# The order of the tiles in SBUF in a fused mLSTM, MLP and expert-mixture kernel

## The chip, the core and the metric

The program runs on one core of one Trainium2 chip. The metric is the device time of one execution in microseconds (us). A kernel's time is the median of several runs.

## The reference, cut to what matters

Three layers follow one another. 1,536 tokens (2 batches of 768) pass through an attention-like recurrence over 8 heads of 40 features, then through an MLP, then through 4 experts whose outputs are mixed by probabilities for each token.

```python
# layer 1: gated recurrence per head, y = o * (C q) / max(|n q|, 1)
x = attn_out.transpose(0, 2, 1, 3).reshape(1536, 320)
# layer 2: MLP, d_ff = 2048
h = x @ w_in
x = (h - np.tanh(h)) @ w_out
# layer 3: 4 experts, d_ff = 1024 each
for e in range(4):
    h = np.maximum(x @ w1[e], 0.0)
    out += p[:, e:e + 1] * (h @ w2[e])
```

## The kernel before

Each float32 operand of the two big layers is split into a high part of the type float32r and a low part, the rest that the high part leaves out. A product is then three matmuls (high by high, high by low, low by high). So the tiles come in pairs: `x_hi` and `x_lo` hold the activations with features on the partitions, `g_hi` and `g_lo` hold the hidden activations, and `w_all` holds both parts of 8 pieces of weights. `w_raw` is a ring of 3 slots in which the weights arrive by DMA. ScalarE writes the high parts, VectorE the low parts of activations, GpSimd the low parts of weights.

The main loop has 64 + 96 steps. Each step `m` does `up(m)` (features of x to a tile of 128 hidden features) and then `down(m - 1)`, so that TensorE works on one step while ScalarE and VectorE turn the result of the other into `g_hi` and `g_lo`.

- Steps 0 to 63 are the MLP: 4 groups of tokens with 256, 384, 384 and 512 tokens, 16 hidden tiles each. `up` is 8 matmuls (lines 1124 to 1128) with `w_all` stationary and `x_hi` or `x_lo` moving. `down_rows` is 8 matmuls (lines 1145 to 1147, twice, then 1153 and 1154) with `w_all` stationary and `g_hi` or `g_lo` moving. The attention of later chunks of 128 tokens is laid between these steps (lines 963 to 1011), with its own tiles: `feat` and `tok` (rings of inputs), `zb`, `fb`, `wa`, `state`, `spare`, and parts of `arena`. Chunks 5 to 11 send their sums through DRAM and read them back.
- Steps 64 to 159 are the experts: 4 experts, 3 groups of 512 tokens, 8 hidden tiles. `up` is the same 8 matmuls of 512 columns. `down_tokens` is 12 matmuls (lines 1174 to 1176, four times) of 320 columns, with `g_hi` or `g_lo` stationary and `w_all` moving. `out_acc`, a view of `arena`, gathers the mixed output, and 12 DMAs store it.

Tiles are placed in the order in which the code names them, one behind another, each at a multiple of 32 bytes. The build puts `w_all` at byte 16,512 of each partition, which is 258 times 64. All sizes up to `probs` are whole multiples of 64 bytes. `tok` has 3 x 968 floats, 11,616 bytes, which is 181.5 times 64. So in the kernel before, everything named behind `tok` begins 32 bytes past a multiple of 64: `feat` at 169,632, `zb`, `wa`, `fb`, `state`, `arena` at 197,600, `g_tmp` at 212,960, `g_hi` at 217,056, `g_lo` at 221,152 and `tails` at 225,248. The tiles ahead of it (`w_all`, `w_raw`, `x_hi` at 123,520, `x_lo`, `spare`, `ident`, `probs`, and `tok` itself at 158,016) begin at multiples of 64.

Of the kernel before, what the change touches and what calls it, by code (L numbers as in the profile page):

```python
# [6 lines left out]
F32R = mybir.dt.float32r  # L7
# [4 lines left out]
P = 128  # L12
BATCH, HEADS, SEQ, HD = 2, 8, 768, 40
D = HEADS * HD
TAIL = D - 2 * P
CH = P
CPB = SEQ // CH
STEPS = BATCH * CPB
TOK = BATCH * SEQ
HDE = HD + 1  # L20
QUAD = 4
PAIRS = HEADS // 2
# [4 lines left out]
RING = 3  # L27
# [19 lines left out]
ROWS = 64 + CPB * HEADS  # L47
# [15 lines left out]
GRP = 4 * CH  # L63
# [39 lines left out]
def mlstm_mlp_experts(nc, gates_d, tok_d, feat_d, w_d, probs_d, out_d):  # L103
    ctx = ExitStack()
    with ctx:
        def sb(name, shape, dt=F32):
            return ctx.enter_context(nc.sbuf_tensor(name, shape, dt))
# [3 lines left out]

        w_all = sb("w_all", [P, WARM, 2 * PIECE], F32R)
        w_raw = sb("w_raw", [P, RING, PIECE])


        x_hi = sb("x_hi", [P, 3, TOK], F32R)
        x_lo = sb("x_lo", [P, 2, TOK], F32R)
        spare = sb("spare", [P, 6 * P])  # L120
        yt = spare[:, 0:2 * D].rearrange("p (r d) -> p r d", d=D)

# [1 line left out]
        ident = sb("ident", [P, P])  # L124
        probs = sb("probs", [P, STEPS, EXPERTS])

        tok = sb("tok", [P, RING, 3 * D + HEADS])
        feat = sb("feat", [P, RING, 2 * PAIRS * CH])

        zb = sb("zb", [P, 2, HEADS, CH])  # L130

        wa = sb("wa", [P, 3, ROWS])

        fb = sb("fb", [P, PAIRS, CH])

        state = sb("state", [P, BATCH, PAIRS, 2, 64])

        dn = state[:, 0, 0, 1, 64 - HEADS:64]

        arena = sb("arena", [P, STEPS * D])  # L140
        dwork = arena[:, 0:1024].rearrange("p (q c) -> p q c", q=2)
        pwork = arena[:, 1024:3072].rearrange("p (r q c) -> p r q c", r=2, q=2)
        wv = arena[:, 3072:3728].rearrange("p (r h e) -> p r h e", r=2, e=HDE)
        beta = arena[:, 3728:3728 + ROWS]
        out_acc = arena[:, 0:STEPS * D].rearrange("p (n d) -> p n d", d=D)
        g_tmp = sb("g_tmp", [P, 2, GRP])
        g_hi = sb("g_hi", [P, 2, GRP], F32R)
        g_lo = sb("g_lo", [P, 2, GRP], F32R)
        tails = sb("tails", [P, 2, GRP])
        tail = tails[0:TAIL, :, :]  # L150


        early = g_tmp[0:ROWS, :, :].rearrange("p b c -> p (b c)")
# [1087 lines left out]
```

## Time and profile before

| | us |
|---|---|
| median of 3 runs | 598.75 |
| lowest and highest run | 597.57, 599.56 |
| the profiled execution, its whole time | 597.8 |
| its span, first to last instruction | 596.1 |
| TensorE busy in the span | 586.9 |
| VectorE, ScalarE, GpSimd busy | 237.2, 201.0, 104.1 |

The rows further down come from the profiled execution. Its whole time is 1.7 us more than its span. A matmul's recorded duration includes the time in which it overlaps with the next one, so the pace of TensorE is read from the distances between the starts of matmuls, not from durations.

### The profile page before, as it was taken

To read this page: it belongs to the slowest core of one execution; us is meant where nothing else is said; L and a number is where in the kernel's file an instruction comes from. 1 tells how busy PE (TensorE), PEld (TensorE's weight loads), DVE (VectorE), ACT (ScalarE), POOL (GpSimd) and SP (SyncE) were. 2 spreads that over 40 slices of the span, in tenths; PEclk is the share of its full clock that TensorE was granted. 3 is DMA by queue.
4 is the path that set the end of the run, shared out by engine and by line. 5 is a ranking of instruction groups with operands and counts; after the bars stand their busy time and mean duration, and the time that the engine had idled before them with its cause. 6 is when DMAs were issued, how large, how long until landed. Compare 5 with 4: busy or idle time off the path is not lost.

```text
span 596.1 us, 8943 instructions
## 1 busy us (share of the span) xinstructions
PE 586.9 (98%) x3660; PEld 531.9 (89%) x3660; DVE 237.2 (40%) x474; ACT 201.0 (34%) x396; POOL 104.1 (17%) x75
## 2 busy tenths in 40 slices
PE   8999999999999999999999999999999999999998
PEld 7899999989988888899999999999999999999997
DVE  6566757676655333413132313131323131323222
ACT  5675645555534444611113311113311111111111
POOL 3868201111000244420003400004400000000000
PEclk9999999999999999999999999999999999999999
DMA  6978544554220133210001210001000000001011
GB/s 252 347 241 279 221 111 134 169 158 112 58 50 27 38 98 104 93 58 0 1 1 48 98 49 1 1 1 48 1 0 1 2 0 1 1 0 45 1 44 46
DMA packets 35343, 43.84 MB, mean 74 GB/s; under 512 B 18670, under 2 KB 27878, under 8 KB 35302
## 3 DMA queue, kind: packets, MB, share of 16 engines
q1 hardware_dynamic: 35302, 43.26, 22.6%
q8 instruction: 29, 0.48, 0.3%
q14 instruction: 12, 0.10, 0.1%
HBM read 38.85 MB, written 4.40 MB: 73 GB/s over the span
## 4 chain that ended last, share of the span: by engine, by line
PE 90%; DVE 5%; issue 1%; DMA 1%; SPq 1%; ACT 1%; DVEq 0%
PE bank L1125 10%; PE bank L1126 10%; PE bank L1124 10%; PE bank L1175 9%; PE bank L1176 9%; PE bank L1174 9%; PE bank L1128 5%; PE bank L1127 5%; PE bank L1145 4%; PE bank L1147 3%; PE bank L1146 3%; PE bank L1153 1%; PE bank L1154 1%; PE bank L963 1%; PE bank L974 1%
## 5 line engine op out<-in xcount | busy, mean ns | idle before, releaser
L940 DVE SCALAR_TENSOR_TENSOR g_lo<-bank,g_hi 128x512 fp32r<-128x512 f32 x96 | 66.3, 691 | 254.2 <-ACT g_hi L659 254.2
L659 ACT ACTIVATE g_hi<-bank 128x512 fp32r<-128x512 f32 x96 | 57.5, 599 | 270.5 <-PE bank L1128 270.4
L1175 PE MATMUL bank<-w_all,g_hi 128*128 128x320 f32 x384 | 118.8, 309 | 0.0
L1176 PE MATMUL bank<-w_all,g_lo 128*128 128x320 f32 x384 | 118.6, 309 | 0.0
L1124 PE MATMUL bank<-x_hi,w_all 128*128 128x512 f32 (+2 forms) x318 | 117.2, 369 | 1.3 <-DVE x_hi L841 1.3
L1174 PE MATMUL bank<-w_all,g_hi 128*128 128x320 f32 x384 | 118.5, 309 | 0.0
L1126 PE MATMUL bank<-x_hi,w_all 128*128 128x512 f32 (+2 forms) x318 | 118.4, 372 | 0.0
L1125 PE MATMUL bank<-x_lo,w_all 128*128 128x512 f32 (+2 forms) x318 | 118.3, 372 | 0.0
L480 POOL TENSOR_TENSOR w_all<-w_raw,w_all 128x1408 fp32r<-128x1408 f32 x16 | 51.6, 3227 | 232.6 <-ACT w_all L542 232.6
L1175 PEld LDWEIGHTS bank<-w_all,g_hi 128*128 128x128 f32 x384 | 72.2, 188 | 3.8
L1174 PEld LDWEIGHTS bank<-w_all,g_hi 128*128 128x128 f32 x384 | 72.2, 188 | 3.7
L1176 PEld LDWEIGHTS bank<-w_all,g_lo 128*128 128x128 f32 x384 | 72.2, 188 | 0.0
L1126 PEld LDWEIGHTS bank<-x_hi,w_all 128*128 128x128 f32 x318 | 59.7, 188 | 8.9
L1124 PEld LDWEIGHTS bank<-x_hi,w_all 128*128 128x128 f32 x318 | 59.7, 188 | 7.5 <-DVE x_hi L841 2.0
L1125 PEld LDWEIGHTS bank<-x_lo,w_all 128*128 128x128 f32 x318 | 59.6, 188 | 6.0
L907 DVE TENSOR_TENSOR bank<-bank,g_tmp 128x384 f32<-128x384 f32 (+2 forms) x64 | 36.1, 564 | 66.0 <-ACT g_tmp L633 65.1
L1128 PE MATMUL bank<-x_hi,w_all 128*128 128x512 f32 (+2 forms) x160 | 59.0, 369 | 0.0
L1127 PE MATMUL bank<-x_hi,w_all 128*128 128x512 f32 (+2 forms) x160 | 58.9, 368 | 0.0
L633 ACT ACTIVATE g_tmp<-bank 128x384 f32<-128x384 f32 (+2 forms) x64 | 31.3, 490 | 70.8 <-PE bank L1128 70.2
L1145 PE MATMUL bank<-g_hi,w_all 128*128 128x384 f32 (+2 forms) x128 | 46.0, 359 | 2.9 <-DVE g_lo L921 2.8
L921 DVE TENSOR_TENSOR g_lo<-bank,g_hi 128x384 fp32r<-128x384 f32 (+2 forms) x64 | 35.4, 553 | 22.5 <-ACT g_hi L651 22.0
L1147 PE MATMUL bank<-g_hi,w_all 128*128 128x384 f32 (+2 forms) x128 | 43.4, 339 | 0.0
(134 smaller groups left out, 644.0 us busy)
## 6 DMA issues: line engine op xcount, KB each, us to landing
w_raw<-in_w SPq DMA_DIRECT2D x24, 704.0 KB, 4.1
feat<-in_feat SPq DMA_DIRECT2D x12, 512.0 KB, 4.7
tok<-in_tok SPq DMA_DIRECT2D x12, 484.0 KB, 5.6
zb<-z SPq DMA_DIRECT2D x10, 512.0 KB, 4.5
out<-arena SPq DMA_DIRECT2D x12, 160.0 KB, 1.9
spare<-xg SPq DMA_DIRECT2D x7, 256.0 KB, 2.6
fb<-f SPq DMA_DIRECT2D x14, 80.0 KB
xg<-feat SPq DMA_DIRECT2D x14, 80.0 KB
```

The lines of the kernel that those rows point to most:

```text
L659: A(g_hi[:, b, 0:N], h_ps[b][:, 0:N], ACT.Relu).then_inc(ghi_ready, 1)
L940: V.scalar_tensor_tensor(g_lo[:, b, 0:N], h_ps[b][:, 0:N], 0.0, g_hi[:, b, 0:N].bitcast(F32), ALU.max, ALU.subtract).then_inc(g_ready, 1)
L1124: mm(h, up_part(m, 0, k), x_hi[:, k, c], start=k == 0, stop=False)
L1125: mm(h, up_part(m, 0, k), x_lo[:, k, c], start=False, stop=False)
L1126: mm(h, up_part(m, 1, k), x_hi[:, k, c], start=False, stop=False)
L1127: mm(h, up_part(m, 0, 2), x_hi[:, 2, c], start=False, stop=False)
L1128: mm(h, up_part(m, 1, 2), x_hi[:, 2, c], start=False, stop=True).then_inc(h_ready, 1)
L1145: mm(out, high_w, high_g, start=first, stop=False)
L1147: mm(out, low_w, high_g, start=False, stop=stop)
L1174: mm(out, g_hi[:, b, t], high_w, start=first, stop=False)
L1175: mm(out, g_hi[:, b, t], low_w, start=False, stop=False)
L1176: last = mm(out, g_lo[:, b, t], high_w, start=False, stop=stop)
```

## The change

The calls that make the tiles are put in another order. `w_all`, `w_raw`, `x_hi` and `x_lo` stay where they are. Behind them come `g_tmp`, `g_hi`, `g_lo`, `tails` and `arena`, then `zb`, `feat`, `fb`, `state`, `spare`, `ident`, `probs` and `wa`, and `tok` is last. No instruction is added, taken away or moved; only the addresses of operands differ. From the sizes, `g_tmp` now begins at 154,240, `g_hi` at 158,336, `g_lo` at 162,432, `tails` at 166,528, `arena` at 170,624, `zb` at 185,984, `feat` at 194,176, `fb` at 206,464, `state` at 208,512, `spare` at 212,608, `ident` at 215,680, `probs` at 216,192, `wa` at 216,384 and `tok` at 217,728. All of these are multiples of 64.

```diff
         x_hi = sb("x_hi", [P, 3, TOK], F32R)
         x_lo = sb("x_lo", [P, 2, TOK], F32R)
-        spare = sb("spare", [P, 6 * P])
-        ident = sb("ident", [P, P])
-        probs = sb("probs", [P, STEPS, EXPERTS])
-        tok = sb("tok", [P, RING, 3 * D + HEADS])
-        feat = sb("feat", [P, RING, 2 * PAIRS * CH])
-        zb = sb("zb", [P, 2, HEADS, CH])
-        wa = sb("wa", [P, 3, ROWS])
-        fb = sb("fb", [P, PAIRS, CH])
-        state = sb("state", [P, BATCH, PAIRS, 2, 64])
+        g_tmp = sb("g_tmp", [P, 2, GRP])
+        g_hi = sb("g_hi", [P, 2, GRP], F32R)
+        g_lo = sb("g_lo", [P, 2, GRP], F32R)
+        tails = sb("tails", [P, 2, GRP])
         arena = sb("arena", [P, STEPS * D])
-        g_tmp = sb("g_tmp", [P, 2, GRP])
-        g_hi = sb("g_hi", [P, 2, GRP], F32R)
-        g_lo = sb("g_lo", [P, 2, GRP], F32R)
-        tails = sb("tails", [P, 2, GRP])
+        zb = sb("zb", [P, 2, HEADS, CH])
+        feat = sb("feat", [P, RING, 2 * PAIRS * CH])
+        fb = sb("fb", [P, PAIRS, CH])
+        state = sb("state", [P, BATCH, PAIRS, 2, 64])
+        spare = sb("spare", [P, 6 * P])
+        ident = sb("ident", [P, P])
+        probs = sb("probs", [P, STEPS, EXPERTS])
+        wa = sb("wa", [P, 3, ROWS])
+        tok = sb("tok", [P, RING, 3 * D + HEADS])
```

## Rows read from the trace of the kernel before

**Rows 1.** The page: TensorE's busy share, its granted clock, the chain by engine.

```profile
PE 586.9 (98%) x3660; PEld 531.9 (89%) x3660; DVE 237.2 (40%) x474; ACT 201.0 (34%) x396; POOL 104.1 (17%) x75
...
PEclk9999999999999999999999999999999999999999
...
PE 90%; DVE 5%; issue 1%; DMA 1%; SPq 1%; ACT 1%; DVEq 0%
```

**Rows 2.** Busy time by stretches: start, MLP without attention, experts, end.

```profile
core 0: us, PE busy (x) PEld busy (x) DVE busy (x) ACT busy (x) POOL busy (x), PEclk, DMA share, GB/s
0.00:19.50 19.50, 17.49 (x117) 14.67 (x117) 13.19 (x40) 10.08 (x20) 9.34 (x19) 0.91 0.72 265
...
214.00:249.70 35.70, 35.70 (x155) 28.84 (x155) 13.21 (x19) 18.06 (x25) 15.52 (x5) 1.00 0.31 101
...
400.00:592.00 192.00, 192.00 (x1070) 174.16 (x1069) 47.94 (x79) 36.84 (x57) 12.90 (x4) 1.00 0.03 11
592.00:596.10 4.10, 1.11 (x8) 0.85 (x6) 1.76 (x4) 0.00 (x0) 0.00 (x0) 1.00 0.47 160
```

**Rows 3.** TensorE's waits from 20 to 250 us: total, times, longest.

```profile
PE bank L1145 <- DVE g_lo L921: 2.8, 7, 1.3
PE bank L1124 <- DVE x_hi L841: 1.3, 2, 0.9
```

**Rows 4.** Timeline of TensorE, MLP steps of 256, 384, 512 columns: start, duration.

```profile
23.14 0.28 PE L1124 MATMUL bank<-x_hi,w_all 128*128 128x256 f32 x1
...
24.09 0.28 PE L1145 MATMUL bank<-g_hi,w_all 128*128 128x256 f32 x1
...
25.05 0.28 PE L1124 MATMUL bank<-x_hi,w_all 128*128 128x256 f32 x1
...
182.60 0.34 PE L1124 MATMUL bank<-x_hi,w_all 128*128 128x384 f32 x1
...
184.01 0.34 PE L1145 MATMUL bank<-g_hi,w_all 128*128 128x384 f32 x1
...
185.25 0.34 PE L1154 MATMUL bank<-g_lo,w_all 128*128 128x384 f32 x1
...
241.74 0.39 PE L1124 MATMUL bank<-x_hi,w_all 128*128 128x512 f32 x1
...
243.59 0.40 PE L1145 MATMUL bank<-g_hi,w_all 128*128 128x512 f32 x1
...
245.46 0.39 PE L1124 MATMUL bank<-x_hi,w_all 128*128 128x512 f32 x1
```

**Rows 5.** The same timeline, one expert step.

```profile
400.39 0.39 PE L1124 MATMUL bank<-x_hi,w_all 128*128 128x512 f32 x1
...
402.23 0.31 PE L1174 MATMUL bank<-w_all,g_hi 128*128 128x320 f32 x1
...
403.99 0.39 PE L1124 MATMUL bank<-x_hi,w_all 128*128 128x512 f32 x1
```

**Rows 6.** Groups of TensorE by shape: count, busy us, mean ns of one.

```profile
L1126 PE MATMUL bank<-x_hi,w_all 128*128 128x512 f32 x224 | 88.5, 395 | 0.0
...
L1145 PE MATMUL bank<-g_hi,w_all 128*128 128x512 f32 x32 | 12.8, 399 | 0.1
...
L1174 PE MATMUL bank<-w_all,g_hi 128*128 128x320 f32 x384 | 118.5, 309 | 0.0
```

**Rows 7.** Groups of VectorE, then of ScalarE, by shape (512 columns).

```profile
L921 DVE TENSOR_TENSOR g_lo<-bank,g_hi 128x512 fp32r<-128x512 f32 x16 | 11.1, 692 | 10.1 <-ACT g_hi L651 10.0
...
L876 DVE TENSOR_TENSOR x_lo<-bank,x_hi 128x512 fp32r<-128x512 f32 x2 | 1.3, 686 | 1.2 <-ACT x_hi L618 1.2
```

```profile
L651 ACT ACTIVATE g_hi<-bank 128x512 fp32r<-128x512 f32 x16 | 9.6, 600 | 11.6 <-DVE bank L907 11.5
...
L618 ACT ACTIVATE x_hi<-bank 128x512 fp32r<-128x512 f32 x2 | 1.1, 596 | 1.3 <-PE bank L1154 1.3
```

**Rows 8.** The page: DMA issues, count, KB each, us to landing.

```profile
w_raw<-in_w SPq DMA_DIRECT2D x24, 704.0 KB, 4.1
feat<-in_feat SPq DMA_DIRECT2D x12, 512.0 KB, 4.7
```

More of the change, by code:

```diff
@@ L119, in mlstm_mlp_experts @@
         x_lo = sb("x_lo", [P, 2, TOK], F32R)
-        spare = sb("spare", [P, 6 * P])
-        yt = spare[:, 0:2 * D].rearrange("p (r d) -> p r d", d=D)
-        xg = spare[:, :].rearrange("p (k g t) -> p k g t", k=3, g=2)
-        ident = sb("ident", [P, P])
-        probs = sb("probs", [P, STEPS, EXPERTS])
-        tok = sb("tok", [P, RING, 3 * D + HEADS])
-        feat = sb("feat", [P, RING, 2 * PAIRS * CH])
-        zb = sb("zb", [P, 2, HEADS, CH])
-        wa = sb("wa", [P, 3, ROWS])
-        fb = sb("fb", [P, PAIRS, CH])
-        state = sb("state", [P, BATCH, PAIRS, 2, 64])
-        dn = state[:, 0, 0, 1, 64 - HEADS:64]
+        g_tmp = sb("g_tmp", [P, 2, GRP])
+        g_hi = sb("g_hi", [P, 2, GRP], F32R)
+        g_lo = sb("g_lo", [P, 2, GRP], F32R)
+        tails = sb("tails", [P, 2, GRP])
+        tail = tails[0:TAIL, :, :]
         arena = sb("arena", [P, STEPS * D])
@@ L145, in mlstm_mlp_experts @@
         out_acc = arena[:, 0:STEPS * D].rearrange("p (n d) -> p n d", d=D)
-        g_tmp = sb("g_tmp", [P, 2, GRP])
-        g_hi = sb("g_hi", [P, 2, GRP], F32R)
-        g_lo = sb("g_lo", [P, 2, GRP], F32R)
-        tails = sb("tails", [P, 2, GRP])
-        tail = tails[0:TAIL, :, :]
+        zb = sb("zb", [P, 2, HEADS, CH])
+        feat = sb("feat", [P, RING, 2 * PAIRS * CH])
+        fb = sb("fb", [P, PAIRS, CH])
+        state = sb("state", [P, BATCH, PAIRS, 2, 64])
+        dn = state[:, 0, 0, 1, 64 - HEADS:64]
+        spare = sb("spare", [P, 6 * P])
+        yt = spare[:, 0:2 * D].rearrange("p (r d) -> p r d", d=D)
+        xg = spare[:, :].rearrange("p (k g t) -> p k g t", k=3, g=2)
+        ident = sb("ident", [P, P])
+        probs = sb("probs", [P, STEPS, EXPERTS])
+        wa = sb("wa", [P, 3, ROWS])
+        tok = sb("tok", [P, RING, 3 * D + HEADS])
         early = g_tmp[0:ROWS, :, :].rearrange("p b c -> p (b c)")
```

## The prediction

> **What bounds the kernel now.** I read the page first, then the busy time by stretches, then the waits of TensorE, and last single steps on the timeline. The page says that TensorE (PE) is busy for 586.9 of 596.1 us and that the chain which ended last is 90% TensorE; its clock is granted in full [rows 1]. The stretches say where the missing 9.2 us lie: 19.50 - 17.49 = 2.0 us in the start, 4.10 - 1.11 = 3.0 us in the end, none in the MLP without attention, none in the experts [rows 2]. What is left, 4.2 us, lies between 20 and 250 us, and two waits for VectorE make up 2.8 + 1.3 = 4.1 us of it [rows 3]. So the time is a sum of matmul paces, and the change can act in four places: the pace of a matmul whose moving operand is displaced, the pace of one whose stationary operand is, the small instructions of the other engines that lie on the chain, and DMAs.
>
> A busy TensorE hides its own losses, so the paces must come from starts. A step of the experts takes 403.99 - 400.39 = 3.60 us, of which 8 matmuls of `up` take 1.84 us (230 ns each for 512 columns) and 12 of `down_tokens` take 1.76 us (146.7 ns each for 320 columns) [rows 5]. At 2.4 GHz, the upper of the clock's two levels, 512 columns are 213.3 ns and 320 are 133.3 ns. So there are 17 and 13 ns on top, and if alignment were behind them, 96 steps of 20 matmuls would have about 27 us to give. The question is therefore whether the operands that are at 32 bytes past a multiple of 64 pay more than those that are not. The kernel before has both kinds side by side.
>
> **The change, part by part.**
>
> Moving operand. In `up` both operands are already at multiples of 64 (`w_all` stationary, `x_hi` and `x_lo` moving) and don't move. In `down_rows` the stationary one is `w_all`, and the moving ones are `g_hi` and `g_lo`, displaced by 32 bytes. The two stand in one step with equal columns. At 512 columns: 8 of `up` from 241.74 to 243.59, 231.3 ns each; 8 of `down_rows` to 245.46, 233.8 ns each, 2.5 more. At 384: 182.60 to 184.01, 176.3 ns; then 7 distances in 1.24 us, 177.1 ns, 0.8 more. At 256: 0.95 us, 118.8 ns; then 0.96 us, 120.0 ns, 1.2 more [rows 4]. Starts are given to 10 ns, so that each of these means is known to 1 ns or so. There are 16 tiles x 8 = 128 such matmuls in a group of tokens: 128 at 512 columns, 256 at 384, 128 at 256. If all of the difference is alignment, the change gives back 128 x 2.5 + 256 x 0.8 + 128 x 1.2 = 0.32 + 0.20 + 0.15 = 0.7 us. Recorded durations give a wider bound: 399 against 395 ns at 512 columns [rows 6], 4 ns, and with 4 ns for all 512 matmuls that is 2.0 us. The lower bound is nothing, since `down_rows` also differs in the banks that it writes. I take half of the 0.7 us, 0.35 us, because the differences are of the size of the rounding.
>
> Stationary operand. In `down_tokens` the moving operand is `w_all`, in place, and the stationary ones are `g_hi` and `g_lo`, displaced. No aligned matmul of 320 columns exists, so I compare with the line through the aligned ones: halfway between 118.8 ns at 256 and 176.3 ns at 384 is 147.5 ns [rows 4], against 146.7 ns measured [rows 5]. The displaced operand pays nothing; read the other way, putting it in place could cost 0.8 ns on each of 96 x 12 = 1,152 matmuls, 0.9 us. The other bound is the rounding of the comparison, 1 ns in favour of the change, 1.2 us. I take 0. The loads of the stationary operand are busy for 174.16 us of 192.00 beside the matmuls [rows 2], so a shorter load alone would lie beside other work; if it were longer than the matmul ahead of it, TensorE would pay, and that is the loss above.
>
> The 13 to 17 ns on top of each matmul are thus paid by aligned operands too. The change doesn't reach them. Where it could have been worth 27 us, nothing in these rows says that it is worth more than 2.
>
> The rule of the Trainium skill that bears on this is in "SBUF — State Buffer", under Specifications: SBUF is read in lines of 16 bytes. An address 32 bytes past a multiple of 64 is at the start of such a line, and so by that rule the first two terms are exactly 0, against the 0.35 us that I take from the rows. No row here shows the size of a line. Without this rule the sum is as worked out above.
>
> Small instructions. VectorE's `g_lo` (displaced) takes 692 ns against 686 ns for `x_lo` (in place) with the same operation and shape; ScalarE's `g_hi` takes 600 against 596 ns [rows 7]. That is 0.9% and 0.7%. Elsewhere it is hidden: in the experts TensorE never waits [rows 2], and the copies end long before their step does. It counts only where these engines are on the chain: 5% of 596.1 us is 30 us of VectorE, 1% is 6 us of ScalarE [rows 1]. 0.9% of 30 is 0.27 us, 0.7% of 6 is 0.04 us. Upper bound 0.3 us, lower bound 0. Two pairs with two instances on one side are thin, and I take 0.1 us.
>
> DMAs. `feat`, `zb`, `fb`, `state` and `arena` are moved to multiples of 64; `w_raw` and `tok` begin at such addresses before and after. The trace has `w_raw`, in place, landing 704 KB in 4.1 us, and `feat`, displaced, 512 KB in 4.7 us [rows 8]. Per byte `feat` is slower by (4.7/512)/(4.1/704) = 1.6, but these are times from issue to landing, with what is queued ahead in them, and much of `feat` is loaded in the crowded first 65 us. Most of these loads are chunks ahead of their use. What they could give is capped by the waits of TensorE that the attention causes, 4.1 us [rows 3], plus some of the 2.0 us of the start [rows 2]. The other bound is 0. Since TensorE's waits name VectorE, and the DMAs are 1% of the chain (6 us) [rows 1], I take 0.
>
> The Trainium skill, "DMA: Bandwidth & Descriptors", § How a descriptor splits into AXI transactions, says that a transfer's pieces begin at multiples of 256 bytes and that an odd start costs beats of 32 bytes. `feat` begins 160 bytes past a multiple of 256 before the change and 128 past one after it, so by that rule a row of 4,096 bytes costs 133 beats before and 132 after, an estimate of 1% of a hidden transfer, which would leave the sum unchanged. No row shows it.
>
> **The sum**, against the profiled execution: 597.8 - 0.35 - 0 - 0.1 - 0 = 597.35 us. The median of the runs shown is 598.75, 0.95 us above the profiled one, so on that footing it is 598.3 us. A measurement of this kernel can tell a change from none at about 0.3%, which is 1.8 us.
>
> **The rivals.**
>
> *Displaced operands cost more than the step rows show, faster.* For: all three widths put `down_rows` above `up`, and the recorded durations say 4 ns. Full price: 2.0 us of matmuls plus 0.3 us of small instructions is 2.3 us, 596.5 us. Against: 4 ns is only seen at 512 columns, and the starts say 2.5. It decides from 1.8 us on. Chance 0.05.
>
> *The transfers of the attention get shorter, faster.* Seven waits for `g_lo` at L1145 and two for `x_hi` at L1124 go away, 4.1 us at most, so 594.6 us; half of it gives 596.7. For: `feat` and `zb` are read and written by DMA, and chunks 5 to 11 pass through DRAM. Against: VectorE, not DMA, ends the waits. Chance 0.05.
>
> *Stationary and moving operand get in each other's way, slower.* After the change both operands of `down_tokens` start at multiples of 64, before they were 32 bytes apart. If reads of equal phase collide, each of the 1,152 matmuls pays. The point from which it decides is 1.8 us / 1,152 = 1.6 ns each. One cycle at 2.4 GHz for every 16 of the 320 columns, 20 cycles or 8.3 ns, would give 9.6 us, 608.3 us. For: the displaced pair lies 0.8 ns under the aligned line. Against: `up` has both operands at multiples of 64 and all three of its widths lie near one line with the displaced one. Chance 0.05.
>
> *The change doesn't do what it says.* The sizes add up to multiples of 64 for all tiles, so this could only be a tile that matters and was aligned anyway; that is the forecast.
>
> **How the numbers follow.** The forecast, within 0.3% of the time before, has 0.84, the three rivals 0.05 each, and 0.01 stays for a slowdown that I don't see. Faster 0.10, same 0.84, slower 0.06. The likeliest time is 598.3 us. Its own terms reach from 598.75 - 2.0 - 0.3 to 598.75 + 0.9, and the runs themselves spread by 1 us to both sides. The range 596.4 to 600.3 us holds this and the milder ends of the two faster rivals; 594.6 and 608.3 are left out.
>
> **What the profile after would show.** An expert step still of 3.60 us, with 1.84 and 1.76 us in it. A 512-column MLP step of 3.72 us, or 3.70 if the moving operand mattered. `g_lo` at 692 or 686 ns. TensorE's waits from 20 to 250 us at about 4 us. I am wrong if an expert step is off by more than 20 ns (1.8 us over 96 steps), or if the waits fall by 2 us.

## The result and the profile after

The changed kernel takes 595.84 us (median of 20 runs, 593.52 to 599.27), the kernel before 598.49 us (median of 20, 597.47 to 602.86). The ratio is 0.9953, 95% interval 0.994 to 0.9965: it is faster by 0.47%, or 2.65 us. The forecast was 598.3 us in a range from 596.4 to 600.3, and "no change" had 0.84.

The page of the changed kernel (lines of the code are two further down: 1145 is now 1147, 1174 is 1176):

```profile
PE 584.8 (98%) x3660; PEld 531.5 (89%) x3660; DVE 238.3 (40%) x474; ACT 201.0 (34%) x396; POOL 104.0 (17%) x75
...
PE 90%; DVE 6%; ACT 2%; issue 1%; DVEq 0%; ACTq 0%
```

TensorE's waits from 20 to 250 us:

```profile
PE bank L1147 <- DVE g_lo L923: 3.1, 6, 1.3
PE bank L1126 <- DVE x_hi L843: 1.3, 2, 0.9
```

So the waits are what they were [rows 3], 4.4 against 4.1 us. TensorE is busy 2.1 us less: the gain is in the matmuls. Its timeline, in the MLP at 384 columns (the last 8 matmuls of a step), at 512 columns, and in the experts (start, duration):

```profile
184.28 0.33 PE L1147 MATMUL bank<-g_hi,w_all 128*128 128x384 f32 x1
...
185.49 0.34 PE L1156 MATMUL bank<-g_lo,w_all 128*128 128x384 f32 x1
...
240.74 0.39 PE L1126 MATMUL bank<-x_hi,w_all 128*128 128x512 f32 x1
...
242.55 0.39 PE L1147 MATMUL bank<-g_hi,w_all 128*128 128x512 f32 x1
...
244.37 0.39 PE L1126 MATMUL bank<-x_hi,w_all 128*128 128x512 f32 x1
...
400.73 0.30 PE L1176 MATMUL bank<-w_all,g_hi 128*128 128x320 f32 x1
...
402.48 0.39 PE L1126 MATMUL bank<-x_hi,w_all 128*128 128x512 f32 x1
...
404.32 0.30 PE L1176 MATMUL bank<-w_all,g_hi 128*128 128x320 f32 x1
```

Here is the surprise. At 512 columns a step takes 244.37 - 240.74 = 3.63 us, 0.09 less than before [rows 4], and `up` has its part in it: 1.81 us for its 8 matmuls against 1.85, though no operand of `up` was moved relative to the other. `down_rows` takes 1.82 against 1.87 us. Both are at one pace now, 227 ns. At 384 columns, 7 distances take 1.21 us, 172.9 ns, against 177.1. An expert step is 1.75 + 1.84 = 3.59 us. Of the steps of 384 columns, those with no attention between their matmuls took 2.80 to 2.83 us (steps 45 and 46 of the kernel before start at 176.96 and 179.77, step 47 at 182.60 us) and take 2.77 us now (177.34, 180.12, 182.89). At 256 columns there was nothing to gain: a step takes 1.92 us, where it took 1.91.

The small instructions of VectorE did not change, with `g_lo` now in place as `x_lo` is:

```profile
L923 DVE TENSOR_TENSOR g_lo<-bank,g_hi 128x512 fp32r<-128x512 f32 x16 | 11.1, 692 | 10.1 <-ACT g_hi L653 10.0
...
L878 DVE TENSOR_TENSOR x_lo<-bank,x_hi 128x512 fp32r<-128x512 f32 x2 | 1.3, 686 | 1.1 <-ACT x_hi L620 1.1
```

They take 692 and 686 ns, exactly as in [rows 7]: the 6 ns between them were never a matter of place.

To add up where the time went, the starts of `up` at the same steps stand side by side (us):

| | before | after | after - before | gained in between |
|---|---|---|---|---|
| step 16 (MLP, first of 384 columns) | 65.53 | 66.42 | +0.89 | -0.89 (lost) |
| step 48 (MLP, first of 512) | 185.98 | 186.25 | +0.27 | 0.62 |
| step 64 (first of the experts) | 245.46 | 244.37 | -1.09 | 1.36 |
| step 159 (last) | 587.59 | 585.74 | -1.85 | 0.76 |

The profiled execution of the changed kernel starts late. Its first matmuls of the MLP (256 columns) come 210 ns apart, which is the pace of 1.2 GHz, the lower level (256 columns are 213 ns):

```profile
19.61 0.41 PE L1120 MATMUL bank<-x_hi,w_all 128*128 128x256 f32 x1
19.82 0.41 PE L1121 MATMUL bank<-x_hi,w_all 128*128 128x256 f32 x1
```

The stretch before them (the columns are those of [rows 2]):

```profile
0.00:19.50 19.50, 17.73 (x114) 15.02 (x115) 13.36 (x39) 10.20 (x20) 9.07 (x19) 0.86 0.70 264
```

The granted clock of this stretch is 0.86 where before had 0.91 [rows 2]. That differs from execution to execution (below, the same kernel had 1.00). Of the 0.89 us, 0.81 are lost by step 2 (it starts at 23.95 against 23.14 us) and 0.08 in the steps of 256 columns behind it. Without the 0.89 us the three stretches give 0.62 + 1.36 + 0.76 = 2.74 us, beside the 2.65 us between the medians. The 0.62 us of the second stretch are what its 15 steps without attention gained (0.64 us together); the steps with attention vary by more than that from execution to execution (exp_64 below, with the same places in the MLP, needs 120.48 us for this stretch, the changed kernel 119.83, the kernel before 120.45). Of the 0.76 us of the third, 0.14 lie before step 66, where the last `down_rows` of the MLP runs inside step 64.

### The profile page after: what moved, and what is told of

The parts are those of the page before. It is cut to its first block, busy times and chain, and to the rows that moved or that the text cites. A ratio compares the mean times of both kernels' runs of the same rounds, so it can differ in the third digit from the quotient of the medians.

```text
span 594.2 us, 8943 instructions
## 1 busy us (share of the span) xinstructions
PE 584.8 (98%) x3660; PEld 531.5 (89%) x3660; DVE 238.3 (40%) x474; ACT 201.0 (34%) x396; POOL 104.0 (17%) x75
## 4 chain that ended last, share of the span: by engine, by line
PE 90%; DVE 6%; ACT 2%; issue 1%; DVEq 0%; ACTq 0%
PE bank L1126 11%; PE bank L1127 10%; PE bank L1128 10%; PE bank L1178 9%; PE bank L1177 9%; PE bank L1176 9%; PE bank L1130 5%; PE bank L1129 5%; PE bank L1147 4%; PE bank L1149 3%; PE bank L1148 3%; PE bank L1156 1%; PE bank L1155 1%; PE bank L976 1%; PE bank L965 1%
```

## The experiments

In all of them the instructions and their order are those of the changed kernel; what differs is where tiles stand. (g_16 and g_4 also leave out the mixing weights of the last two chunks of tokens, to make room.) The cuts of code that give only names are a shorthand: they list the tiles in the order in which they are made. Where `tok` stands decides: it is the only tile whose size is an odd multiple of 32 bytes, so that what follows it is displaced. "Step at 512" is the mean of 13 MLP steps (start of step 63 less start of step 50), "expert step" the mean of 92 (step 158 less step 66). The shift is that of a tile against `w_all` within 256 bytes; why 256 is found at the end. Every slice that a matmul reads begins a whole number of 256 bytes behind the start of its tile, so that one shift holds for all matmuls of a pair of tiles.

| kernel | tiles against `w_all` | starts of steps 50, 63 | step at 512 | starts of 66, 158 | expert step | ratio to before (95%) |
|---|---|---|---|---|---|---|
| before | g at 96 | 193.37, 241.74 | 3.721 | 252.79, 583.99 | 3.600 | 1 |
| after | g at 0 | 193.59, 240.74 | 3.627 | 251.56, 582.15 | 3.593 | 0.9953 (0.994 to 0.9965) |
| g_only | g at 0, others displaced | 193.93, 241.07 | 3.626 | 251.89, 582.48 | 3.593 | 0.9951 (0.9934 to 0.9968) |
| g_off | g at 96, others in place | 193.82, 242.09 | 3.713 | 253.13, 584.34 | 3.600 | 1.0001 (0.9987 to 1.0014) |
| x_off | x at 96, g at 0 | 194.87, 243.23 | 3.720 | 254.30, 587.34 | 3.620 | 1.0043 (1.0026 to 1.006) |
| all_off | all at 0, but all 32 past a multiple of 64 | 193.64, 240.78 | 3.626 | 251.61, 582.19 | 3.593 | 0.9956 (0.994 to 0.9972) |
| w_off | x and g at 160 | 194.60, 243.33 | 3.748 | 254.46, 588.42 | 3.630 | 1.003 (1.001 to 1.0051) |
| g_64 | g at 192 | 193.45, 241.55 | 3.700 | 252.53, 582.51 | 3.587 | 0.9937 (0.9915 to 0.9958) |
| g_16 | g at 80 | 192.81, 240.39 | 3.660 | 251.29, 583.41 | 3.610 | 0.9993 (0.9973 to 1.0013) |
| g_4 | g at 68 | 193.24, 242.03 | 3.753 | 253.16, 583.74 | 3.593 | 0.9992 (0.9968 to 1.0016) |
| exp_64 | g at 0 in the MLP, 64 in the experts | 194.49, 241.63 | 3.626 | 252.46, 582.43 | 3.587 | 0.9962 (0.9944 to 0.998) |
| after_again | g at 0 | 194.54, 241.69 | 3.627 | 252.51, 583.10 | 3.593 | 0.9965 (0.9952 to 0.9979) |

**Which tiles.** First, `g_hi` and `g_lo` alone, from both sides.

```diff
 # g_only: the order; what is behind tok is displaced
+w_all w_raw x_hi x_lo g_hi g_lo spare ident probs
+tok
+g_tmp tails arena zb feat fb state wa
 # g_off
+w_all w_raw x_hi x_lo g_tmp tails arena zb feat fb state spare ident probs wa
+tok
+g_hi g_lo
```

> Only g_hi and g_lo are put at multiples of 64; g_tmp, tails, arena, zb, feat, fb, state and wa stay 32 bytes past one, as before. Theory A (the loss sits in TensorE's reads of g_hi and g_lo): all of the gain, an MLP step of 512 columns at 3.63 us instead of 3.72, an expert step at 3.593 instead of 3.600, time about 595.9 us where before is 598.5 (ratio 0.9955). Theory B (the gain comes from the other engines and the DMAs, whose tiles were moved too): MLP step 3.72 us, ratio 1.00.

> The kernel after the change, with g_hi and g_lo alone put back to 32 bytes past a multiple of 64. Theory A: the whole loss comes back, MLP step 3.72 us, expert step 3.600 us, ratio to before 1.000. Theory B: stays as the kernel after, MLP step 3.63 us, ratio 0.9955.

Theory A holds on both sides: two tiles in place give the whole gain (0.9951), two tiles displaced take it all back (1.0001). The MLP step of g_off, and its experts:

```profile
193.82 0.39 PE L1116 MATMUL bank<-x_hi,w_all 128*128 128x512 f32 x1
...
242.09 0.39 PE L1116 MATMUL bank<-x_hi,w_all 128*128 128x512 f32 x1
...
253.13 0.39 PE L1116 MATMUL bank<-x_hi,w_all 128*128 128x512 f32 x1
...
584.34 0.39 PE L1116 MATMUL bank<-x_hi,w_all 128*128 128x512 f32 x1
```

(242.09 - 193.82) / 13 = 3.713 us and (584.34 - 253.13) / 92 = 3.600 us. DMAs and the other engines' tiles, all in place here, give nothing that the ratio or the steps show.

**A place of its own, or a place relative to another tile.** Displace the other moving operand, and then everything.

```diff
 # x_off: x_hi and x_lo behind tok
+w_all w_raw g_tmp g_hi g_lo tails arena zb feat fb state spare ident probs wa
+tok
+x_hi x_lo
 # all_off: everything behind tok
+tok
+w_all w_raw x_hi x_lo g_tmp g_hi g_lo tails arena zb feat fb state spare ident probs wa
```

> The kernel after the change, with x_hi and x_lo (moving operands of up in every step) put 32 bytes past a multiple of 64, g_hi and g_lo in place. If a displaced moving operand pays (theory A1), then up pays in all 160 steps: MLP step of 512 columns again about 3.72 us, expert step about 3.65 us (8 matmuls at 7 to 8 ns more, as down_rows paid before), so some 5 us more in the experts and 2.5 us in the MLP, time about 603 us, ratio 1.008. If only a displaced g_hi or g_lo matters, because other engines write them at the same time (theory A2): MLP step 3.63 us, ratio 0.9955.

> The kernel after the change with tok placed first, so that every other tile is 32 bytes past a multiple of 64. If the absolute start of a moving operand counts: up and down_rows both pay, expert step 3.65 us or more, MLP step 3.75 us, ratio 1.008 or more. If what counts is that stationary and moving operand differ in their place within 64 bytes (theory C): they agree here, so MLP step 3.63 us, expert step 3.593 us, ratio 0.9955.

```profile
194.87 0.40 PE L1116 MATMUL bank<-x_hi,w_all 128*128 128x512 f32 x1
...
243.23 0.40 PE L1116 MATMUL bank<-x_hi,w_all 128*128 128x512 f32 x1
...
254.30 0.40 PE L1116 MATMUL bank<-x_hi,w_all 128*128 128x512 f32 x1
...
587.34 0.40 PE L1116 MATMUL bank<-x_hi,w_all 128*128 128x512 f32 x1
```

x_off: 3.720 and 3.620 us. The MLP pays as before, now through `x`, which no engine writes at the time; A2 falls. The experts pay 27 ns for each step against the changed kernel, half of what A1 expected, and the kernel takes 600.64 us where A1 expected about 603. And all_off:

```profile
193.64 0.39 PE L1116 MATMUL bank<-x_hi,w_all 128*128 128x512 f32 x1
...
240.78 0.39 PE L1116 MATMUL bank<-x_hi,w_all 128*128 128x512 f32 x1
...
251.61 0.39 PE L1116 MATMUL bank<-x_hi,w_all 128*128 128x512 f32 x1
...
582.19 0.39 PE L1116 MATMUL bank<-x_hi,w_all 128*128 128x512 f32 x1
```

3.626 and 3.593 us, ratio 0.9956: with every matmul operand 32 bytes past a multiple of 64, the kernel is as fast as with none. The start of a tile at a multiple of 64 is worth nothing by itself. What counts is how tiles stand to one another.

**Stationary against moving, or moving against moving.** `w_all` alone is displaced; in the MLP all moving operands then still stand alike.

```diff
 # w_off: w_all behind tok
+w_raw x_hi x_lo g_tmp g_hi g_lo tails arena zb feat fb state spare ident probs wa
+tok
+w_all
```

> The kernel after the change with w_all alone put 32 bytes past a multiple of 64; x_hi, x_lo, g_hi and g_lo stay in place, so that all moving operands of the MLP still begin alike. Theory C (what counts is whether the stationary operand, which is loaded while the matmul before streams, and the moving one stand alike within 64 bytes): every matmul of the MLP is mismatched, step of 512 columns at 16 x 234 ns = 3.74 us, and up of the experts too, step at 3.62 us, ratio to before about 1.005. Theory C2 (what counts is the jump in place from one moving operand to the next): no loss in the MLP, 3.63 us; in the experts 3.62 us, ratio about 1.001.

```profile
194.60 0.40 PE L1116 MATMUL bank<-x_hi,w_all 128*128 128x512 f32 x1
...
243.33 0.40 PE L1116 MATMUL bank<-x_hi,w_all 128*128 128x512 f32 x1
```

3.748 us, against the 3.74 of theory C and the 3.63 of C2; in the experts 3.630 us, where both expected 3.62. In the MLP at 512 columns the place that matters is that of the stationary operand, which TensorE loads while it streams, against the moving one. With x and g equally off, the 16 matmuls take 3.748 / 16 = 234 ns on average.

**Where in a step the time goes.** The distances from each matmul to the next, as means over the 13 steps from 50 to 62 (ns):

| kernel | `up`, 8 matmuls | `down_rows`, 8 matmuls |
|---|---|---|
| before (g at 96) | 231 231 234 229 232 231 227 227 | 236 234 235 231 240 234 236 232 |
| x_off (x at 96) | 235 234 235 231 240 234 236 232 | 231 231 236 228 232 231 227 227 |
| w_off (both at 160) | 234 or 235 each | 234 or 235 each |
| after (both at 0) | 227 each | 227 each |

The half whose moving tile is displaced pays in all of its matmuls, 65 ns in the kernel before. The other half pays as well, 29 ns, but only in its first six matmuls; the last two are back at 227 ns. In x_off the two halves have changed places. The same fading is seen in the experts of the changed kernel, where all tiles are at 0: after `down_tokens`, `up` takes 231, 236, 228, 232, 231 and then 227 ns three times. So `up` also pays for what ran before it, and that part the change left in the experts (1.84 us for 8 matmuls, as before). What `down_tokens` gained lies mostly in its first two matmuls, 143 and 145 ns where it was 146 and 147; from the third on its mean is 147 ns before and after.

The shift alone doesn't fix the pace. In w_off, two steps of 384 columns without attention, step 19 and step 23, take 2.82 us (81.48 - 78.66) and 2.77 us (96.28 - 93.51) with all tiles in the same place. Nor is 0 the best at every width: g_64, described next, takes 1.87 us for step 2, of 256 columns (25.84 - 23.97), the changed kernel 1.91 (25.86 - 23.95). The starts of steps 19, 20, 23 and 24 in w_off, then of steps 2 and 3 in g_64:

```profile
78.66 0.34 PE L1116 MATMUL bank<-x_hi,w_all 128*128 128x384 f32 x1
...
81.48 0.34 PE L1116 MATMUL bank<-x_hi,w_all 128*128 128x384 f32 x1
...
93.51 0.34 PE L1116 MATMUL bank<-x_hi,w_all 128*128 128x384 f32 x1
...
96.28 0.34 PE L1116 MATMUL bank<-x_hi,w_all 128*128 128x384 f32 x1
```

```profile
23.97 0.28 PE L1116 MATMUL bank<-x_hi,w_all 128*128 128x256 f32 x1
...
25.84 0.28 PE L1116 MATMUL bank<-x_hi,w_all 128*128 128x256 f32 x1
```

**How finely the place counts.** g_64 puts `probs` (192 bytes) ahead of `g_tmp`. Its expectation calls the shift 64 bytes; it is 192, or 64 the other way round within 256.

```diff
 # g_64: probs moved up
-x_lo g_tmp g_hi g_lo tails arena zb feat fb state spare ident probs wa tok
+x_lo probs g_tmp g_hi g_lo tails arena zb feat fb state spare ident wa tok
 # g_16 and g_4: both in one tile, read from its float 4 or 1 on
+g_all = sb("g_all", [P, 4 * GRP + 8], F32R)
+g_hi = g_all[:, 4:4 + 2 * GRP].rearrange("p (b c) -> p b c", b=2)
```

> The kernel after the change with probs (192 bytes) placed ahead of g_tmp, so that g_hi, g_lo and all that follows stand 64 bytes past the place that they share with w_all and x_hi within 256 bytes. If 64 bytes is the unit: no change, MLP step 3.627 us, expert step 3.593 us, ratio to before 0.9955. If the unit is 128 or 256 bytes: MLP step between 3.66 and 3.72 us, ratio 0.998 to 1.000.

> g_hi and g_lo begin 16 bytes past a multiple of 64, w_all and x in place. (The mixing weights of the last two chunks of tokens are replaced by those of another chunk, to free 32 bytes.) If any displacement within 64 bytes costs: MLP step of 512 columns near 3.72 us, expert step 3.600 us. If the unit is a line of 16 bytes: 3.627 and 3.593 us, as with no displacement.

> g_hi and g_lo begin 4 bytes past a multiple of 64, w_all and x in place. (The mixing weights of the last two chunks of tokens are replaced by those of another chunk, to free 32 bytes.) If the cost is one more fetched line of 64 bytes for each operand: the full cost at 4 bytes already, MLP step near 3.72 us. If it grows with the displacement: a step of 3.64 us, an eighth of the loss at 32 bytes.

```profile
193.45 0.40 PE L1116 MATMUL bank<-x_hi,w_all 128*128 128x512 f32 x1
...
241.55 0.39 PE L1116 MATMUL bank<-x_hi,w_all 128*128 128x512 f32 x1
...
252.53 0.40 PE L1116 MATMUL bank<-x_hi,w_all 128*128 128x512 f32 x1
...
582.51 0.40 PE L1116 MATMUL bank<-x_hi,w_all 128*128 128x512 f32 x1
```

All tiles of g_64 are at multiples of 64, and its MLP step is 3.700 us: 64 bytes is not the unit. In the sweeps below a shift of 192 gives both numbers again, and a shift of 80 gives again the 3.610 us of g_16 in the experts. Its expert step, 3.587 us, is better than the 3.593 of the changed kernel. Its whole time was expected at a ratio of 0.998 to 1.000 and came out at 0.9937, which by the two intervals can't be told from the changed kernel. The stretches say why: against the changed kernel it gains 0.39 us from step 2 to 16 (256 columns) and 0.53 us from step 64 to 159, and loses 1.07 us from step 48 to 64. g_16 and g_4 stand at shifts of 80 and 68, as their tile begins at 64. They gave 3.660 and 3.753 us in the MLP. That fits no expectation: the displacement that was 12 bytes smaller cost more, so the price neither grows evenly nor is one fixed price for a line that is straddled.

To find the unit, two kernels, sweep1 and sweep2, change the shift every few steps. The memory of `feat` is free from step 48 on. Each kernel was run once, and only its steps are used:

```diff
+with nc.sbuf_tensor("room", [P, RING * 2 * PAIRS * CH], F32R) as room:
+    pass                       # feat is placed over it
 feat = sb("feat", [P, RING, 2 * PAIRS * CH])
+def g_of(m, low):
+    if m < 48:
+        return (g_lo if low else g_hi)[:, m % 2, :]
+    shift = OWN_ROWS[(m - 48) // 4] if m < L1_STEPS else OWN[(m - L1_STEPS) // TPU]
+    at = (2 * low + m % 2) * 768 + shift // 4
+    return room[:, at:at + GRP]
```

> The kernel after the change; from step 48 on, g_hi and g_lo stand in the memory of feat, which is free by then, and their place is shifted by a number of bytes that changes every 8 steps in the experts (0, 32, 64, 96, 128, 160, 192, 256, 320, 384, 448, 0) and every 4 steps in the last group of the MLP (128, 256, 64, 0). A shift of 0 stands like w_all and x_hi within 512 bytes. If 64 bytes were the unit, all shifts by multiples of 64 would give 3.627 and 3.593 us; the run before this one already had 3.700 and 3.587 at 192. If the unit is 128: 128 and 256 give 3.627 us in the MLP, and 64 gives 3.70. If it is 256: 256 gives 3.627 and 128 does not. If it is 512: neither does.

> The same with other shifts: 512, 1024, 16, 48, 80, 112, 224, 288, 352, 416, 480, 0 in the experts, and 384, 192, 32, 512 in the last group of the MLP. If the unit is 512 or less: 512 gives 3.627 us in the MLP, 512 and 1024 give 3.593 in the experts; 192 repeats 3.70 and 32 repeats 3.72 (3.713 measured with g_hi and g_lo alone displaced). If the unit is 256: 384 gives what 128 gave.

The step at each shift, once it has settled: in the experts the mean of six steps (the third to the eighth of a shift), in the MLP the mean of the last two of four (starts are given to 10 ns, so these means are good to 5 ns). Rows of sweep1 for 256 and 64 bytes in the MLP, then for 64 and 128 bytes in the experts:

```profile
208.42 0.39 PE L1139 MATMUL bank<-x_hi,w_all 128*128 128x512 f32 x1
...
215.67 0.39 PE L1139 MATMUL bank<-x_hi,w_all 128*128 128x512 f32 x1
...
222.96 0.39 PE L1139 MATMUL bank<-x_hi,w_all 128*128 128x512 f32 x1
...
230.31 0.39 PE L1139 MATMUL bank<-x_hi,w_all 128*128 128x512 f32 x1
...
309.73 0.40 PE L1139 MATMUL bank<-x_hi,w_all 128*128 128x512 f32 x1
...
331.25 0.40 PE L1139 MATMUL bank<-x_hi,w_all 128*128 128x512 f32 x1
...
367.24 0.39 PE L1139 MATMUL bank<-x_hi,w_all 128*128 128x512 f32 x1
...
388.88 0.39 PE L1139 MATMUL bank<-x_hi,w_all 128*128 128x512 f32 x1
```

(215.67 - 208.42) / 2 = 3.625 us at 256, (230.31 - 222.96) / 2 = 3.675 at 64; (331.25 - 309.73) / 6 = 3.587 at 64, (388.88 - 367.24) / 6 = 3.607 at 128. All of them:

| shift within 256 | MLP step at 512, us | expert step, us (shifts tried) |
|---|---|---|
| 0 | 3.625 (0), 3.625 (256), 3.630 (512) | 3.593 (0, 256, 512, 1024) |
| 16 | | 3.587 (16) |
| 32 | 3.720 | 3.613 (32, 288) |
| 48 | | 3.593 (48) |
| 64 | 3.675 | 3.587 (64, 320) |
| 80 | | 3.610 (80) |
| 96 | | 3.600 (96), 3.602 (352) |
| 112 | | 3.600 (112) |
| 128 | 3.690 (128), 3.700 (384) | 3.607 (128, 384) |
| 160 | | 3.600 (160, 416) |
| 192 | 3.700 | 3.587 (192, 448) |
| 224 | | 3.607 (224, 480) |

In the experts, every shift repeats what the same shift plus 256 gives, eight pairs in all, to 2 ns; the unit is 256 bytes. In the MLP only 0, 256 and 512 give 3.627 us; the one other pair there, 128 and 384, differs by 10 ns. The change worked because with its order `g_hi` stands 141,824 bytes behind `w_all`, which is 554 times 256; that it is a multiple of 64 would not have been enough.

**A version from the sweeps.** 0 is best in the MLP at 512 columns, 16, 64 and 192 in the experts. exp_64 has 0 and 64, with the changed kernel once more beside it:

```diff
+    if m < L1_STEPS:
+        return (g_lo if low else g_hi)[:, m % 2, :]
+    at = (2 * low + m % 2) * 768 + 64 // 4
```

> The kernel after the change; in the experts g_hi and g_lo stand in the memory of feat, 64 bytes past the place of w_all and x_hi within 256 bytes, in the MLP they stay at 0. From the sweeps: MLP step of 512 columns 3.627 us, expert step 3.587 us, so 96 x 6.7 ns = 0.64 us less than after the change, about 595.2 us, ratio to before 0.994. If the sweep's numbers hold only beside their neighbours: expert step 3.593 us, ratio 0.9955.

> The changed kernel once more beside exp_64 on the same chip: MLP step 3.627 us, expert step 3.593 us, ratio to before 0.9955. The steps come out the same to a nanosecond, if they follow from addresses; the start of the kernel, up to the first matmul of the MLP, may differ by 0.5 us with TensorE's clock.

The steps came as expected, 3.626 and 3.587 us, 92 steps of the experts in 329.97 us against 330.59. The times of the whole kernels are 595.2 and 596.12 us, with ratios of 0.9962 and 0.9965, which can't be told apart: 0.6 us is 0.1%. The ratio 0.994 that was expected lies just outside the interval of exp_64 (0.9944 to 0.998); only the steps show this gain.

## Why the prediction was wrong

**The bound** was right: the time is a sum of matmul paces, and the waits stayed at 4 us.

**The moving operand** is the step that failed: "The two stand in one step with equal columns", and hence the difference between `down_rows` and `up` was taken for the whole price, 2.5 ns at 512 columns, 0.7 us in all, and halved to 0.35. `up` was no undisturbed control. Its own pace in that step was 231.3 ns [rows 4], and fell to 227 ns (1.813 / 8) when only the operands of its neighbour were moved. The price at 512 columns is 94 ns for a step (3.7207 - 3.6266 us), 65 ns of it in `down_rows`, 8 ns for each matmul, and 29 ns in the first six matmuls of `up`. The 2.5 ns themselves were rounding in part: over 13 steps the two halves take 1.843 and 1.878 us, 4.4 ns a matmul apart. Measured over the stretches it was 1.36 us at 512 columns and 0.62 us at 384, together 2.0 us where I had 0.35. At 256 columns, where 0.15 us had been counted, nothing came back. Why `up` goes on paying for six matmuls after its neighbour, no run shows.

The number that could have warned me was in view: I wrote that 512 columns cost 17 ns more than at 2.4 GHz (and 320 columns 13 ns; for all 96 steps that is 28 us, not 27), concluded from aligned operands paying it too that "the change doesn't reach them", and never asked whether "aligned" meant a tile's own place or its place against another.

**The stationary operand** was taken at 0, with bounds from a loss of 0.9 to a gain of 1.2 us. The expert steps gained 6.7 ns each, 0.64 us over 96, inside the bounds. Of the stationary term only the settled pace was right: 147 ns a matmul before and after. The gain came at the turn from `up` to `down_tokens`, which the term had no place for. The line drawn through `up` at 256 and 384 columns was one through disturbed paces; halfway between 119.8 and 173.4 ns, the paces of the changed kernel, is 146.6 ns. The sweeps also show that in the experts a shift of 0 is not the best: 16, 64 and 192 are 6.7 ns a step better.

**The rival** with the faster sign had the right place, and its full price of 2.3 us was near the 2.74 us of the stretches, but it had 0.05. That the price came near was luck in part: it held 0.3 us for small instructions, which gave 0, and nothing for `up` and for the experts. The rival of slower matmuls (both operands of `down_tokens` at equal phase) was the right kind of mechanism, one between the two operands, and had the sign wrong here: equal phase is the best of the shifts tried in the MLP at 512 columns, and in the experts 6.7 ns a step better than what was before.

**Small instructions**: 0.1 us taken, 0 found, 692 and 686 ns as before. **DMAs**: 0 taken, and none found; g_only has `feat`, `zb`, `fb`, `state` and `arena` displaced and all of the gain.

**The rules of the Trainium skill.** "SBUF — State Buffer", Specifications, has lines of 16 bytes; by that rule I had an exact 0 for the two matmul terms. The runs differ: shifts of 16, 32 and 64 bytes are all whole lines and give 3.587, 3.613 and 3.587 us in the experts. "TensorE: Matmul & The Clock Gate", in its step-by-step account of LDWEIGHTS, says that loading the next weights takes no SBUF bandwidth from the running matmul. By that rule the place of the weights would be free. The measured paces differ: with the same instructions, 227 or 234 ns for 512 columns by the place of `w_all` alone (the changed kernel against w_off). Whether it is bandwidth that is lost, no run shows.

What stays open is the mechanism. Shown is that the pace depends on the stationary and the moving tile's relative place, and in the experts that 256 bytes is the unit. That two reads of TensorE meet in one part of SBUF would fit it, but no run sees such a meeting. g_off and before have the same shift of 96 and yet 3.713 and 3.721 us in the MLP, and w_off has two paces at 384 columns, so the shift doesn't settle everything.

## What to carry to other kernels

Where TensorE sets the time with float32r operands, look at the relative place of stationary and moving tiles within 256 bytes, and try a few at each width: here it moved a step of 16 matmuls of 512 columns between 3.63 and 3.75 us, with no instruction changed, while at 256 columns 192 was better than 0. An edit that "aligns" tiles may work for another reason than its name says; displace everything together, and the two reasons separate. And a control inside the same pipelined loop isn't one until something shows that it doesn't change with the thing it is compared to.

## What the runs showed of the hardware

The pace of a float32r matmul with its own weight load, when all tiles stand at a shift of 0 and the widths don't alternate, is 226.7 ns at 512 columns (3.627 / 16), 173.4 ns at 384 ((182.89 - 177.34) / 32) and 119.8 ns at 256 (steps 2, 6, 10 and 13, 7.67 us for 64 matmuls). Each is 13 ns above the columns at 2.4 GHz (213.3, 160 and 106.7), and so is the settled 146.7 ns of the 320 columns in the experts.

Steps are the same to a nanosecond between the two executions of the changed kernel that were profiled (3.627 and 3.593 us in both); what spreads the times (593.5 to 599.3 us for one kernel) lies elsewhere. The changed kernel's second profile has TensorE's clock at 1.00 in the first 19.5 us (0.86 in the first) and reaches step 16 at 64.41 us instead of 66.42, but then needs 122.79 us to step 48 (187.20 - 64.41) where the first needed 119.83. Its chain and its timeline there:

```profile
105.27 4.03 DMA nq<-feat
109.32 2.46 DMA state<-nq
...
113.99 0.45 PE bank L1147
```

```profile
113.99 0.45 PE L1147 MATMUL bank<-g_hi,w_all 128*128 128x384 f32 x1 [2.31 <-DVE g_lo L923]
...
115.15 0.52 PE L1148 MATMUL bank<-g_lo,w_all 128*128 128x384 f32 x1
115.47 0.52 PE L1149 MATMUL bank<-g_hi,w_all 128*128 128x384 f32 x1
```

A DMA of a few KB through DRAM took 4.03 us, TensorE stood idle for 2.31 us, and then its 384 columns came 320 ns apart: the lower clock level of 1.2 GHz, for some 3 us (the granted clock from 66 to 119 us is 0.97, and 1.00 in the first profile). In the range of a third of a per cent, one such wait hides or feigns the change; the steps, read from starts, do not.
